# Attention, soft MoE and a gated FFN on one core: tokens stored by tile, a ring of four quarter-size transpose buffers, broadcasts of 1/rms inside the last loop

## The reference

```python
attn_out = softmax(scale * mean_pool2(q) @ k.T) @ v          # 4 batches, 8 heads, 576 pooled queries, 1152 keys, d=64
x = attn_out -> (2304 tokens, 512)
# soft MoE: 8 experts, 4 slots each (32 slots), F = 1024
logits = x @ phi
d = softmax over the tokens;  slot_input = d.T @ x
slot_out[e] = relu(slot_input[e] @ w1[e]) @ w2[e]
c = softmax over the slots;   x = c @ slot_out
# gated FFN, d_ff = 1536
rms = sqrt(mean(x * x, -1) + 1e-6);  xn = x / rms * rms_g
g = xn @ w_gate;  val = xn @ w_val
out = (g * sigmoid(g) * val) @ w_out
```

## Time and profile before

| | us |
|---|---|
| three timed runs | 803.42, 804.03, 807.4 |
| the profiled execution | 807.56 |
| its span, first to last instruction | 805.6 |
| attention block | 0 to 539.5 |
| token transposes and logits | 539.8 to 553.1 |
| softmax over tokens, slots, experts | 553.1 to 603 |
| weight folding and 1/rms | 603 to 625 |
| last loop | 625 to 805 |

### The profile page before, as it was taken

One profiled execution on the slowest core, in us unless ns is written; L12 is line 12 of the kernel. 1 busy time (PEld: TensorE's weight loads), 2 busy tenths in 40 slices (PEclk: granted clock), 3 DMA queues, 4 the chain that ended last, 5 costly groups with the idle time before them and its releaser, 6 DMA issues. The chain is left out here.

```text
span 805.6 us, 16312 instructions
## 1 busy us (share of the span) xinstructions
PE 786.8 (98%) x5286; PEld 585.6 (73%) x5286; DVE 500.0 (62%) x967; ACT 460.9 (57%) x873; POOL 181.3 (23%) x243
## 2 busy tenths in 40 slices
PE   7999999999999999999999999989998999999997
PEld 7777777777777777777777777766344888888876
DVE  6766667666666676666756666644325566666665
ACT  5676676676766667666767676642123454434333
POOL 6351331522414325133152240000002330000000
PEclk9999999999999999999999999999998899999999
DMA  8539747365383463744836518586997001010010
GB/s 229 124 88 289 202 104 180 81 150 119 90 201 82 123 157 78 175 103 102 188 74 148 122 34 239 219 290 227 401 400 303 0 1 53 1 52 21 33 52 27
DMA packets 83032, 112.02 MB, mean 139 GB/s; under 512 B 45361, under 2 KB 47409, under 8 KB 82481
## 3 DMA queue, kind: packets, MB, share of 16 engines
q1 hardware_dynamic: 82832, 111.24, 48.7%
q10 hardware_dynamic: 160, 0.26, 0.1%
HBM read 71.37 MB, written 4.72 MB: 94 GB/s over the span
## 5 line engine op out<-in xcount | busy, mean ns | idle before, releaser
L579 PE MATMUL scores<-k_stack,q_stack 128*128 128x384 f32 x960 | 275.1, 376 | 2.8 <-DVE q_stack L796 2.4
L766 ACT COPY pt<-tbank 128x384 f32<-128x384 f32 x288 | 138.2, 480 | 152.8 <-PE tbank L516 152.7
L516 PE MATMUL tbank<-ident,probs 128*128 128x128 f32 x1296 | 219.5, 278 | 0.4 <-ACT probs L738 0.3
L516 PEld LDWEIGHTS tbank<-ident,probs 128*128 128x128 f32 x1296 | 156.5, 140 | 67.8 <-issue 41.9
L738 ACT ACTIVATE probs<-scores,neg_max 128x1152 f32<-128x1152 f32 x144 | 175.9, 1222 | 7.4 <-DVE neg_max L836 3.0
L612 PE MATMUL obank<-pt,v_in 128*64 128x320 f32 (+1 forms) x1152 | 167.3, 417 | 0.9 <-ACT o_t L753 0.9
L832 DVE TENSOR_REDUCE row_max<-scores 128x1 f32<-128x384 f32 x144 | 80.1, 556 | 117.0 <-PE scores L579 115.5
L579 PEld LDWEIGHTS scores<-k_stack,q_stack 128*128 128x128 f32 x960 | 147.8, 191 | 3.8 <-ACT k_stack L378 2.6
L825 DVE TENSOR_REDUCE row_max<-scores 128x1 f32<-128x768 f32 x144 | 136.6, 948 | 2.2 <-PE scores L579 1.6
L612 PEld LDWEIGHTS obank<-pt,v_in 128*64 128x64 f32 x1152 | 72.0, 136 | 58.1 <-issue 25.8
L887 DVE COPY pt<-tbank 128x384 f32<-128x384 f32 x144 | 80.2, 557 | 36.8 <-PE tbank L516 34.1
(11 more groups left out here) (217 smaller groups left out, 702.7 us busy)
## 6 DMA issues: line engine op xcount, KB each, us to landing
weights<-in_moe_w SPq DMA_DIRECT2D x7, 2048.0 KB, 11.4
v_in<-in_v SPq DMA_DIRECT2D x16, 576.0 KB, 4.0
k_in<-in_k SPq DMA_DIRECT2D x30, 288.0 KB, 4.9
k_stack<-k_hi SPq DMA_DIRECT2D x30, 288.0 KB, 3.6
k_stack<-k_lo SPq DMA_DIRECT2D x30, 288.0 KB, 3.6
q_in<-in_q SPq DMA_DIRECT2D x14, 512.0 KB, 5.1
slots_of_four<-in_moe_w SPq DMA_DIRECT2D x12, 512.0 KB, 11.2
q_stack<-q_hi SPq DMA_DIRECT2D x30, 144.0 KB, 3.3
```

What stands on the lines that cost most here:

```text
L516: last = nc.tensor.transpose(tbank[:, bank, cols], src, ident[0:rows, 0:rows])
L579: last = nc.tensor.matmul(scores[:, bank, 0:CH], q_stack[at.par][:, h, order, cols], k_stack[at.par][:, h, keys], start=(x == 0), stop=(x ...
L766: nc.scalar.copy(pt_out(at, e), pt_from(at, e)).then_inc(out_by_act, 1)
```

## The change

What the program does after it, part by part:

- `x_nat` is stored by tile: all pairs' columns of token tile 0, then of tile 1, and so on.
- The transpose jobs are one feature group of one tile with its four batches (20 jobs, four transposes each). `xt` is a ring of four quarter-size buffers. PE makes the transposes of job n, then the four logit matmuls of job n-3.
- `w_third` lies outside the transpose buffers for its first two experts; that half (1 MB) is issued at the end of the attention block. The third expert's part is issued after the logits, the fourth after the slots.
- `w_second` covers tiles 0 and 1 of `x_nat` alone and is issued once `z` has read these (`z_step`).
- In the folding stage, `share(0,0)` takes the place of a filler matmul before the yt product; the transposed 1/rms and the first broadcast come before the last two shares; value(0,0) and value(0,1) are issued as soon as their pieces of `w_low` are copied; ACT makes the pieces 1, 5, 2, 6, 7 and DVE 0, 4, 3.
- The four later broadcasts of 1/rms stand in the last loop's tiles 1 to 4 of chunk 0, in the PSUM bank of the next value product, which is therefore made at the end of the tile. ACT copies all of them.
- The two small copies `tail_inv` move from the folding stage on DVE to tile 6 of the loop.

```diff
@@ attention block, SP
         sp.wait_ge(group_ready, s_groups.upto(NPAIR - 1, 1))
         sp.dma_start(mem.w1_first[:], mem.w1_v[4:8, :, 0, :].rearrange("e p f -> p e f")).then_inc(mem.w1_first_in, 16)
+        sp.dma_start(mem.w1_third[:, 0:2, :], mem.w1_v[4:6, :, 2, :].rearrange("e p f -> p e f")).then_inc(mem.w1_third_in, 16)
...
-    xt = [mem.sb(f"xt{n}", [P, KT, B, P], FP32) for n in range(2)]
+    xt = mem.sb("xt", [P, 4, B, P], FP32)
...
+    xt_jobs = [(i, c) for i in range(NI) for c in range(KT)]
...
     def slots_sync(sp):
-        sp.wait_ge(lt_step, NI)
-        sp.dma_start(w1_next[2][:, 0:3, :], mem.w1_v[4:7, :, 2, :].rearrange("e p f -> p e f")).then_inc(w1_in[2], 16)
-        sp.wait_ge(z_ready, 1)
+        sp.wait_ge(lt_step, len(xt_jobs))
+        sp.dma_start(w1_next[2][:, 2, :], mem.w1_v[6, :, 2, :]).then_inc(w1_in[2], 16)
+        sp.wait_ge(z_step, 1)
         sp.dma_start(w1_next[1], mem.w1_v[4:8, :, 1, :].rearrange("e p f -> p e f")).then_inc(w1_in[1], 16)
...
-        token_transposes(0)
-        for i in range(1, NI):
-            token_transposes(i)
-            logits(i - 1)
-        logits(NF)
+        for n in range(len(xt_jobs)):
+            token_transposes(n)
+            if n >= 3:
+                logits(n - 3)
+        for n in range(len(xt_jobs) - 3, len(xt_jobs)):
+            logits(n)
...
+            if i == 1:
+                last.then_inc(z_step, 1)
...
-            out_bank = banks[:, INV_BANK[n], 0:width]
+            out_bank = gv_ps[:, n % 2, 1, 0:width]
...
-        keep_clock(1)
+        pe.wait_ge(st_out, NG + 1)
+        share(0, 0)
...
         for n in range(CHUNKS):
             for f in range(NFT):
-                if f + 2 < NFT:
+                spread_at = n == 0 and 1 <= f <= B
+                if spread_at:
+                    gate(n, f + 2)
+                    broadcast_inverse(f)
+                elif f + 2 < NFT:
                     gate(n, f + 2)
                     value(n, f + 2)
...
+                if spread_at:
+                    pe.wait_ge(inv_out, f + 1)
+                    value(n, f + 2)
...
                 if k == 0:
+                    share_out(6)
                     share_out(7)
-                    inverse_out(4)
+                if n == 0 and 1 <= f <= B:
+                    inverse_out(f)
                 if n == 0 and f + 1 < NFT:
                     wo_high((f + 1,))
```

More of the change, by code:

```diff
@@ L1054, in logits @@
-        def logits(i):
-            if i == 0:
-                pe.wait_ge(small_in, 32)
-            done = (jobs_of(i)[-1] + 1) // 2
-            pe.wait_ge(xt_out_a, done)
-            pe.wait_ge(xt_out_v, done)
-            rows = rows_of(i)
-            for c in range(KT):
-                for b in range(B):
-                    last = nc.tensor.matmul(lt_ps[32 * b:32 * b + 32, P * i:P * i + rows], phi_sb[:, c, :],
-                                            xt[i % 2][:, c, b, 0:rows],
-                                            start=(c == 0), stop=(c == KT - 1), tile_position=(0, 32 * b))
-            last.then_inc(lt_step, 1)
@@ new lines, in logits @@
+        def logits(n):
+            i, c = xt_jobs[n]
+            rows = rows_of(i)
+            if n == 0:
+                pe.wait_ge(small_in, 32)
+            pe.wait_ge(xt_out_v if n % 2 else xt_out_a, n // 2 + 1)
+            for b in range(B):
+                last = nc.tensor.matmul(lt_ps[32 * b:32 * b + 32, P * i:P * i + rows], phi_sb[:, c, :],
+                                        xt[:, n % 4, b, 0:rows],
+                                        start=(c == 0), stop=(c == KT - 1), tile_position=(0, 32 * b))
+            last.then_inc(lt_step, 1)
@@ L1074, in keep_busy @@
+        for n in range(len(xt_jobs)):
[4 more added lines that the diff above has]
+            logits(n)
         def keep_busy():
[L1075 removed]
+            nc.tensor.matmul(banks[:, NTB - 1, :], ident[:], x_nat[:, 0, 0:NF * P], start=True, stop=True)
         keep_busy()
```

166 lines of the change are left out of this document (72 added, 94 removed).

## The result

| | before | changed |
|---|---|---|
| median of 6 runs each, same chip, us | 804.68 (803.0 to 807.4) | 811.91 (811.38 to 813.44) |
| the profiled execution, us | 807.56 | 813.44 |
| its span, us | 805.6 | 811.4 |

The ratio is 1.0091, with a 95% interval of 1.0069 to 1.0113: slower, by some 7 us. The forecast was 807.5, with 802.0 to 812.8 as its range and 805.8 to 809.2 as the likeliest case's own; the time lies in the first and outside the second.

The account below looks back on a forecast made before the run. PE was taken as the bound, busy 786.8 of 805.6 us. 807.56 + 4.8 + 2.2 - 0.5 - 7.1 + 0.3 = 807.3, or 807.8 from the median; forecast 807.5 us, range 802.0 to 812.8.

Parts of the forecast that it names:

- The base: Profiled execution holds 10.3 us at half clock, costing 4.1 us; two of three timed runs lacked it (median 804.03).
- Part 1: Transposes and logits: the ring of quarter buffers makes PE switch weight forms more often, +4.8 us.
- Rival 3: Transposes and logits: the switches cost nothing extra, giving 802.7 us; chance 0.15.
- Part 2: Seam: one more DMA ahead of the barrier holds SP on a full queue while every engine stands, +2.2 us.
- Rival 4: Seam: the half of w_third is taken without a stop, giving 805.3 us; chance 0.10.
- Rival 1: Transposes: the granted clock falls to 0.50 somewhere from 538 to 555 us, costing 5.1, giving 812.6; chance 0.15.
- Part 3: Loads behind the barrier: all later ones come 2.8 us earlier, value weights 2.3 earlier; -0.5 us at PE.
- Part 4: Folding stage up to the loop's first w_out product: reached 8.0 us sooner, some 2 of it the slow clock.
- rival 2: Folding stage: the clock still falls as in the profiled run, costing 4, giving 811.5 us; chance 0.13.
- Part 5: Last loop: broadcasts and ACT's copy chain make five tiles take 18.9 us against 18.1; -7.1 together with Part 4.
- Part 6: Loop's tile 6: tail_inv's two small copies lie beside POOL's operation, +0.3 us.
- The sum from the median: Whole kernel from 804.03 us, only 3.0 of the 7.1 gain counted: 804.03 + 4.8 + 2.2 - 0.5 - 3.0 + 0.3 = 807.8.

Follow-up runs that it names:

- e4: The kernel before with only the change's new folding stage and last loop; storage, transposes and loads stay as before: 804.12 us, 0.9979 of the kernel before.
- e11: The changed kernel with 512 KB of w_third issued ahead of the barrier instead of 1 MB, the other 512 KB right behind it: 810.50 us.
- e2: The changed kernel with PE making the transposes of two jobs, then the logits of the two jobs before: 807.83 us.
- e1: The changed kernel with the early half of w_third issued as SP's first instruction behind the barrier, not ahead of it: 807.26 us.
- e5: The kernel of e3, with the DMA of w_second waiting again until all of z is done: 805.45 us.
- e3: The changed kernel with the early half of w_third behind the barrier and transposes and logits in pairs of jobs: 805.31 us.
- e8: The changed kernel run again, unedited, beside other kernels: 810.72 us, 1.0070 of the kernel before.
- e9: The kernel of e4, with the broadcasts' products contracting over 128 rows instead of 20, the added rows multiplied by zeros: 803.28 us.
- e12: The kernel of e10, with tail_inv moved to the second batch's third tile, where POOL has no operation beside it: 802.07 us.
- e6: The kernel of e4, with ACT copying each broadcast behind the next tile's Silu in chunk 0: 803.93 us.
- e10: The kernel of e9, with ACT copying each broadcast behind the next tile's Silu in chunk 0: 802.25 us.

## Why the prediction was right or wrong

The forecast said 807.3 from the profiled execution, which became 813.44: 6.1 us are missing. Attention's end, +0.6, is chance. The rest, by the prediction's parts:

**What bounds the kernel: right. The base: the guess that two of three timed runs lacked the slow stretch can't be tested on those three, but was no rule.** More than half of the later executions of the kernel before have a mean clock that holds such a stretch (47 of 85, see e4), and their median is 805.6 to 805.8, not 804.03. The other thirteen profiles say nothing on this, since all but the changed kernel's first (3.4 us) lack the stretch and none is of the old folding stage.

**Part 1, the ring, +4.8: mechanism right, size 0.9 too large.** It cost 3.9 at full clock (13.25 to 17.13): 26 more switches of 0.15, where I had counted 0.16 to 0.19 and some streaming. The working has two slips besides: 3.65 us over 32 transposes is 0.114 and not 0.109, and its own terms (1.89, 0.37, 12.0, 3.1, 0.9) add up to 18.3 and not 18.1. Rival 3, switches free, fell. The Trainium skill (TensorE: Matmul & The Clock Gate, "What overlaps and what doesn't") lets loads overlap only with other row groups; here loads of one form lie 0.23 us apart under 0.39 us matmuls of the same rows, so they do overlap, and what doesn't is a load of another form.

**Part 2, the DMA, +2.2: right,** 2.31, for a reason only half right. I took the 2.5 us from the bytes; e11 shows that the bytes don't set it. Rival 4 fell.

**Rival 1, the clock falls in the transposes: it happened,** and the forecast's "granted clock 1.00 from 538 to 660" is the step that failed. It fell in all five profiles in which the DMA stood ahead of the barrier (PE had stood for 2.7 to 3.7 us), and in none of the nine where PE had stood for 1.34 us. I had set its price at 5.1 us, by the one long stretch in the earlier trace rows; it was 1.6 (18.69 - 17.13), 1.4 (e2) and 2.7 (e11). I had argued against it with the clock at the seam of before, after a wait of 1.3 us. That row said nothing about a wait of 3.65. I had both numbers and treated two terms, the wait and the clock, as independent, although in all five profiles the one came with the other, and in e1 both went.

**Part 3, the earlier loads: failed.** 2.3 us earlier at the value weights, beside the 0.5 at the last W2 piece, were predicted; measured were 0.5 on average over seven profiles, between -0.4 and 1.6 in a single one (numbers under e5), and 0.6 in e3 against e5. The wait at the last W2 piece, gone in the profile, is back with 0.79 us in e8. The failed step is "After that the queue had no pause", and with it "So all later loads come 2.8 us earlier". The 401 GB/s of the earlier trace rows are of a queue in which w_second was still moving when PE freed the next buffers, 2.0 us after the first W1 product. That moment does not move with w_second. Issued earlier, w_second has landed 2.6 us after the product, and the queue falls to 290 and 313 GB/s for the 6 us in which the next loads get under way.

**Part 4, the folding stage, -8.0: half.** From the last high part to the first w_out product 5.2 us, predicted 5.1: each step of that sum held (the first piece runs beside the scaling, so it does not count). But the high part was to come 48.4 us after W1 (612.3 - 563.44, less part 3's 0.5) and came after 52.2. Of these 3.8, 0.9 is the second fall of the clock (e8 lacks it: rival 2, a part of its price). The rest is the weights of part 3: the last value weights were to land 47.2 us after W1 and landed after 50.2.

**Part 5, the loop, 18.9 us for five tiles: the number fair (19.5), the reason wrong.** The chain through ACT's copy does exist: e9, where PE's gaps are gone, takes 18.97, where the prediction's sum was 18.9. That both sums agree to 0.1 us is in part luck: the prediction had 3.85 us for such a tile, and e9's tiles alternate between 4.08 and 3.76. In the changed kernel a slower thing lay over it, two switches a tile between 128 and 20 rows, 0.4 us. I had priced the broadcasts' products at 0.45 a tile from their streaming, with the price of a change of form already in hand from the earlier trace rows, and did not look at the form of their weights.

**Part 6, tail_inv, +0.3: right in kind,** 0.5 by the stretch behind the sixth tile, and e12 takes it back.

Together: ring -0.9, its clock +1.6, seam +0.1, parts 3 and 4 +4.0 (0.5 and 8.0 predicted, 4.5 measured), loop +0.6, tail +0.2, attention +0.6: 6.2, 0.1 of it by rounding. The largest miss is a gain that did not come.

The sum from the median put the gain of parts 4 and 5 at full clock at 3.0. With the prediction's own 4.1 for the slow stretch, an estimate, the kernel before takes 238.1 us from the first W1 product to the end at full clock (242.2 in its profile); e4 takes 238.3. So nothing of the 3.0 came: about 4.0 us were won between the last high part and the loop, 3.6 lost in the loop's first tiles and 0.5 at tail_inv.

The time of 811.9 lies in the stated range, near its upper end and near the 812.6 of rival 1. That nearness is luck: rival 1's event happened at a third of its price, and the rest came from a gain that stayed out.

## What to carry to other kernels

- Before the last barrier of a block, a DMA into a full queue is no free prefetch: it holds its issuing engine, and through the barrier all. Put it behind the barrier, and count the clock into the wait's price.
- Count on PE how often the form of the weights changes (strips against the full array, 20 rows against 128), and pay 0.15 to 0.2 us each time. Padding 20 rows to 128 cost PE nothing here (steps of 0.22 to 0.23 us) and takes both gaps away.
- An early issue helps only as far as the loads behind it can follow. Ask what each of them waits for, and whether that moves too: here the next one stayed at 2.0 us after the first W1 product.
- Before a slow stretch of one profile is counted for or against a kernel, look at the mean clock of all its executions: here 47 of 85 told of it.
- Where an edit of one hold gives nothing, take the trace of that kernel and look for the second hold at the same place before calling the first one false: e6 and e9 gave 0.2 and 0.5 us alone, 1.7 together.

## What the runs showed of the hardware

- A weight load of another form starts near the end of the running matmul's record, also where only the rows differ: steps of 0.54 and 0.11 us where 0.23 and 0.23 is normal, and none of it left with 128 rows everywhere (e10). The Trainium skill (TensorE: Matmul & The Clock Gate, "Step-by-step: what each phase is for") has PE pull loads ahead of running matmuls where the row groups don't conflict or the load goes to the background weight buffer, and says that the row count K doesn't matter for the timing. The first agrees with the loads of one form. The second holds for the load alone (0.18 for 20 rows, 0.19 for 128), not for the step from one count to the other (e9).
- SP stood 2.6 to 3.3 us at one DMA, for 512 KB as for 1 MB, while some 400 GB/s moved; later issues of 0.5 to 2 MB in the same kernels took 0.34 to 0.37 us where there was room.
- After a stand of 2.7 to 3.7 us PE's granted clock was 0.50 for 3.4 us (four profiles) or 6.8 (e11); after one of 1.34 us it stayed at 1.00 (nine profiles).
- Two copies of 64 x 2 values on DVE took 1.46 us beside a POOL operation of 1.29 (1.85 beside 1.80 in the earlier trace rows) and 0.35 without one. The Trainium skill (GPSIMD Engine Reference, "1. Specifications") names contention of GpSimd with DVE instructions in a 2-port perf mode or with two SBUF inputs. The longer times agree with a contention; whether these copies, of one input each, ran in such a mode no run here shows.
